# Layer 1's gate as one Silu activation, and the next pair's squares summed on VectorE, in a Strassen-Winograd attention and two-layer feed-forward kernel

## The reference, cut to what matters

```python
x = attention(q, k, v)                                   # 2304 x 512
xn = x / sqrt(mean(x * x) + 1e-6) * rms_g
g = xn @ w_gate                                          # layer 1, 1536 wide
silu = g * (1.0 / (1.0 + exp(-g)))
x = (silu * (xn @ w_val)) @ w_out
r = maximum(x @ w_in, 0.0)                               # layer 2, 2048 wide
return (r * r) @ w_down
```

## Time and profile before

| what | value |
|---|---|
| median of 3 runs | 911.52 us (909.7 to 911.78) |
| the profiled execution | 909.82 us |
| its span | 907.9 us, 14817 instructions |
| clock of TensorE in it | granted in full in all 40 slices |
| busy PE, PEld | 889.4, 879.4 us |
| busy DVE, ACT, POOL | 609.4, 483.5, 583.8 us |

### The profile page before, as it was taken

The page is one execution under the profiler, slowest core; times in us unless marked ns, Lnnn a source line. Parts: engine busy times, 40 slices in busy tenths (PEclk is TensorE's granted clock), DMA queues, the critical chain, the costliest instruction groups (busy, mean ns, idle before and its releaser), DMA issues.

```text
span 907.9 us, 14817 instructions
## 1 busy us (share of the span) xinstructions
PE 889.4 (98%) x5356; PEld 879.4 (97%) x5356; DVE 609.4 (67%) x861; ACT 483.5 (53%) x872; POOL 583.8 (64%) x568
## 2 busy tenths in 40 slices
PE   6999899999999999999999999999999999999998
PEld 6998899999999999999999999999999999999998
DVE  7777777767867766867776767767377675577222
ACT  4887755654466463555554445544355453455332
POOL 7897749967368977347868448573368553485332
PEclk9999999999999999999999999999999999999999
DMA  9995122211222212222222122222422221420122
GB/s 236 249 230 150 45 64 70 70 53 59 82 65 71 70 53 60 69 80 72 70 70 58 58 88 71 65 58 70 138 72 71 62 67 59 157 70 18 59 70 93
DMA packets 105944, 76.99 MB, mean 85 GB/s; under 512 B 24464, under 2 KB 88976, under 8 KB 105872
## 3 DMA queue, kind: packets, MB, share of 16 engines
q1 hardware_dynamic: 105872, 76.05, 29.1%
HBM read 71.31 MB, written 4.72 MB: 84 GB/s over the span
## 4 chain that ended last, share of the span: by engine, by line
PE 82%; POOL 9%; issue 3%; ACT 3%; DVE 3%; DMA 0%; SPq 0%; POOLq 0%; ACTq 0%; DVEq 0%
PE bank L618 26%; PE bank L620 25%; PE bank L619 25%; PE bank L570 2%; PE bank L593 2%; POOL h L490 1%; POOL sq L529 1%; POOL h L501 1%; POOL w_raw L439 1%; POOL wide L460 1%; POOL w_raw L435 1%; POOL probs L466 1%; PE bank L579 1%; ACT w_hi L816 1%; ACT acts L816 0%
## 5 line engine op out<-in xcount | busy, mean ns | idle before, releaser
L618 PE MATMUL bank<-xc_hi,w_hi 128*128 128x384 f32 x844 | 283.8, 336 | 2.1 <-ACT acts L816 1.0
L620 PE MATMUL bank<-xc_hi,w_lo 128*128 128x384 f32 x844 | 282.1, 334 | 0.0
L619 PE MATMUL bank<-xc_lo,w_hi 128*128 128x384 f32 x844 | 282.1, 334 | 0.0
L618 PE MATMUL bank<-hs_hi,d_hi 128*128 128x384 f32 x672 | 225.3, 335 | 1.9 <-POOL d_lo L508 1.9
L619 PE MATMUL bank<-hs_lo,d_hi 128*128 128x384 f32 x672 | 224.6, 334 | 0.0
L620 PE MATMUL bank<-hs_hi,d_lo 128*128 128x384 f32 x672 | 224.6, 334 | 0.0
L508 POOL TENSOR_TENSOR d_lo<-d_raw,d_hi 128x512 fp32r<-128x512 f32 x84 | 127.1, 1513 | 146.0 <-ACT d_hi L816 146.0
L1219 DVE TENSOR_TENSOR hs_lo<-h,hs_hi 128x768 fp32r<-128x768 f32 x84 | 85.5, 1018 | 126.4 <-ACT hs_hi L816 126.2
L618 PEld LDWEIGHTS bank<-xc_hi,w_hi 128*128 128x128 f32 x844 | 158.4, 188 | 5.8 <-issue 1.8
L619 PEld LDWEIGHTS bank<-xc_lo,w_hi 128*128 128x128 f32 x844 | 158.5, 188 | 0.0
L620 PEld LDWEIGHTS bank<-xc_hi,w_lo 128*128 128x128 f32 x844 | 158.4, 188 | 0.0
(11 more groups left out here) (92 smaller groups left out, 1257.4 us busy)
## 6 DMA issues: line engine op xcount, KB each, us to landing
d_raw<-in_w_down SPq DMA_DIRECT2D x48, 256.0 KB, 2.6
w_raw<-in_w_gate SPq DMA_DIRECT2D x36, 256.0 KB, 2.9
w_raw<-in_w_val SPq DMA_DIRECT2D x72, 128.0 KB, 2.8
d_raw<-in_w_out SPq DMA_DIRECT2D x36, 256.0 KB, 2.6
w_raw<-in_w_in SPq DMA_DIRECT2D x24, 256.0 KB, 2.7
w_raw<-in_w_in SPq DMA_DIRECT2D x48, 128.0 KB, 2.6
k_sb<-in_kT SPq DMA_DIRECT2D x16, 288.0 KB, 4.3
q_diag<-in_qT SPq DMA_DIRECT2D x32, 144.0 KB, 4.9
```

Source lines behind the costliest of these rows:

```text
L618: pe.matmul(ps, w_h, v_h, start=first, stop=False, skip_group_check=joined)
L619: pe.matmul(ps, w_h, v_l, start=False, stop=False, skip_group_check=joined)
L620: return pe.matmul(ps, w_l, v_h, start=False, stop=last, skip_group_check=joined)
```

## The change

In layer 1 ACT writes Silu of the gate where it wrote its sigmoid, so DVE's products ga * sigmoid (L1256, L1171) and `silu_b` (L1206, L1180) go. POOL's `h_a` then multiplies sa with va, and `h_b` waits for ACT. The waits move along: ga waits for act_a_done in place of ha_done, va and `gate_a` now wait for ha_done, and PE's waits on silu_a_done and silu_b_done become waits on act_a_done and act_b_done. The three additions of the next pair's squares leave POOL's list and stand in DVE's, after `low2(u+1)` of steps 4, 5 and 6 of runs 0 and 1.

```diff
@@ gpsimd
                 if first_layer(r):
-                    pool.wait_ge(silu_a_done, u + 1)
+                    pool.wait_ge(act_a_done, u + 1)
                     pool.wait_ge(c21_done, steps_done(u))
-                    nc.gpsimd.tensor_tensor(h_half(n, 0), ga[:], va[:], ALU.mult).then_inc(ha_done, 1)
+                    nc.gpsimd.tensor_tensor(h_half(n, 0), sa[:], va[:], ALU.mult).then_inc(ha_done, 1)
...
-                    pool.wait_ge(silu_b_done, u + 1)
+                    pool.wait_ge(act_b_done, u + 1)
...
-                    if q < PAIRS and s in (4, 5, 6):
-                        k = s - 3
-                        pool.wait_ge(sq_done, 2 * KT + KT * r + k + 1)
-                        if k > 1:
-                            pool.wait_ge(sq_sum, 3 * q + 3 + k - 1)
-                        nc.gpsimd.tensor_tensor(squares[1][0][:], squares[1][0][:], squares[1][k][:],
-                                                ALU.add).then_inc(sq_sum, 1)
@@ tensor
                 elif s >= 2:
-                    if first_layer(r):
-                        pe.wait_ge(silu_b_done, u - 1)
-                    else:
-                        pe.wait_ge(act_b_done, u - 1)
+                    pe.wait_ge(act_b_done, u - 1)
@@ scalar
-                nc.scalar.activation(sbuf_b[:], x, ACT.Sigmoid if first_layer(r) else ACT.Relu).then_inc(act_b_done, 1)
+                nc.scalar.activation(sbuf_b[:], x, ACT.Silu if first_layer(r) else ACT.Relu).then_inc(act_b_done, 1)
...
                 act.wait_ge(c11_done, steps_done(u))
-                if first_layer(r):
-                    act.wait_ge(silu_a_done, u)
-                else:
-                    act.wait_ge(ha_done, u)
-                nc.scalar.activation(sa[:], ga[:], ACT.Sigmoid if first_layer(r) else ACT.Relu).then_inc(act_a_done, 1)
+                act.wait_ge(ha_done, u)
+                nc.scalar.activation(sa[:], ga[:], ACT.Silu if first_layer(r) else ACT.Relu).then_inc(act_a_done, 1)
@@ vector
+            def square_sum(q, k):
+                dve.wait_ge(sq_done, 2 * KT + KT * (q - 1) + k + 1)
+                if k > 1:
+                    dve.wait_ge(sq_sum, 3 * q + 3 + k - 1)
+                nc.vector.tensor_tensor(squares[1][0][:], squares[1][0][:], squares[1][k][:],
+                                        ALU.add).then_inc(sq_sum, 1)
...
-                    if not first and first_layer(r):
-                        silu_b(u - 1, r)
-
                     dve.wait_ge(p2_done, n)
                     dve.wait_ge(t_out, n)
                     if not first or r == 0:
-                        if first_layer(r):
-                            dve.wait_ge(ha_done, u)
-                        else:
-                            dve.wait_ge(act_a_done, u)
+                        dve.wait_ge(act_a_done, u)
                     nc.vector.tensor_tensor(ga[:], Z[:, 0:NT], c_t[:], ALU.add).then_inc(c11_done, 1)
...
+                    if not first and first_layer(r):
+                        dve.wait_ge(ha_done, u)
                     nc.vector.tensor_tensor(va[:], Y[:, 0:NT], c_u[:], ALU.add).then_inc(c21_done, 1)
-                    if first_layer(r):
-                        dve.wait_ge(act_a_done, u + 1)
-                        dve.wait_ge(c11_done, n)
-                        nc.vector.tensor_tensor(ga[:], ga[:], sa[:], ALU.mult).then_inc(silu_a_done, 1)
-                    else:
+                    if not first_layer(r):
...
                     if u + 1 < U0[r + 1]:
                         low2(u + 1)
+                    if r + 1 < PAIRS and s in (4, 5, 6):
+                        square_sum(r + 1, s - 3)
```

More of the change, by code:

```diff
@@ L216, in build @@
         act_a_done, act_b_done = sem("act_a_done"), sem("act_b_done")
-        silu_a_done, silu_b_done = sem("silu_a_done"), sem("silu_b_done")
         ha_done, hb_done = sem("ha_done"), sem("hb_done")
@@ L692, in p1 @@
                 if r == 0 and s == PLAIN:
-                    pe.wait_ge(silu_a_done, 1)
+                    pe.wait_ge(act_a_done, 1)
                 elif r == 0 and s == PLAIN + 1:
@@ L711, in p7 @@
                 elif r == 0:
-                    pe.wait_ge(silu_b_done, 1)
+                    pe.wait_ge(act_b_done, 1)
                 else:
@@ L762, in down @@
                         if k >= 2:
-                            if first_layer(r):
-                                pe.wait_ge(silu_b_done, end + k - 3)
-                            else:
-                                pe.wait_ge(act_b_done, end + k - 3)
+                            pe.wait_ge(act_b_done, end + k - 3)
                     ps = (v_banks(r)[k] if c == 0 else u_banks(r)[B_BANKS[k]])[:, 0:NT]
@@ L789, in _ @@
                         if r == 0:
-                            pe.wait_ge(silu_a_done, 2)
+                            pe.wait_ge(act_a_done, 2)
                             pe.wait_ge(ha_done, 2)
@@ L859, in gate_plain @@
                     act.wait_ge(ga_mm, u + 1)
-                    act.wait_ge(silu_a_done, u)
-                    nc.scalar.activation(sa[:], of[:, 0:NT], ACT.Sigmoid).then_inc(act_a_done, 1)
+                    act.wait_ge(ha_done, u)
+                    nc.scalar.activation(sa[:], of[:, 0:NT], ACT.Silu).then_inc(act_a_done, 1)
                 else:
@@ L864, in gate_plain @@
                     act.wait_ge(hb_done, u)
-                    nc.scalar.activation(sbuf_b[:], of[:, 0:NT], ACT.Sigmoid).then_inc(act_b_done, 1)
+                    nc.scalar.activation(sbuf_b[:], of[:, 0:NT], ACT.Silu).then_inc(act_b_done, 1)
             def x_high(r, b, n=None):
@@ L1166, in gated_a @@
             def gated_a(u):
-                g_ps, v_ps = (bank[0], bank[1]) if u == 0 else (bank[4], bank[5])
+                v_ps = bank[1] if u == 0 else bank[5]
                 dve.wait_ge(act_a_done, u + 1)
-                dve.wait_ge(ha_done, u)
-                nc.vector.tensor_tensor(ga[:], g_ps[:, 0:NT], sa[:], ALU.mult).then_inc(silu_a_done, 1)
-                dve.wait_ge(silu_a_done, u + 1)
                 dve.wait_ge(va_mm, u + 1)
-                nc.vector.tensor_tensor(h_half(u, 0), v_ps[:, 0:NT], ga[:], ALU.mult).then_inc(ha_done, 1)
+                nc.vector.tensor_tensor(h_half(u, 0), v_ps[:, 0:NT], sa[:], ALU.mult).then_inc(ha_done, 1)
             def gated_b(u):
-                g_ps, v_ps = (bank[2], bank[3]) if u == 0 else (bank[6], bank[7])
+                v_ps = bank[3] if u == 0 else bank[7]
                 dve.wait_ge(act_b_done, u + 1)
-                nc.vector.tensor_tensor(sbuf_b[:], g_ps[:, 0:NT], sbuf_b[:], ALU.mult).then_inc(silu_b_done, 1)
-                dve.wait_ge(silu_b_done, u + 1)
                 dve.wait_ge(vb_mm, u + 1)
@@ L1278, in _ @@
                         h_low(m + 1)
-                    if f == 0 and first_layer(r):
-                        silu_b(U0[r + 1] - 1, r)
                     if q < RUNS:
```

## The result

The changed kernel takes 904.26 us (median of 4 runs, 903.6 to 905.16) against 911.46 us of the kernel before (4 runs, 909.7 to 911.78): a ratio of 0.9931, 95% interval 0.9919 to 0.9943, so 5.2 to 7.4 us faster. 906.0 was predicted, with 903.5 to 910.0 as the range. The profiled execution took 904.36 us, its span is 902.6. Repeated later, beside the experiments, the changed kernel took 903.84 us against 909.93, a ratio of 0.9933 (0.992 to 0.9945).

A forecast was written before the change was run, and what follows sets the result against it. PE, busy 98% of the span, was the bound, losing time to late lists; 2.3 + 1.3 + 2.1 less 0.2 for new waits gave 5.5 us, 911.52 - 5.5 = 906.0 us, range 903.5 to 910.0.

The forecast's parts named there:

- The size and the places: PE's lost time in steps 6 to 10 and the last steps: about 6.3 us can be had at most.
- steps 6 and 7: Ahead of the token sums in runs 0 and 1: moving the additions off POOL wins back 2.3 us.
- steps 8 to 10: After the token sums in runs 0 and 1: without POOL's lag 0.65 us each comes back, 1.3 us.
- the down starts: Last step of each layer 1 run: POOL's product starts earlier without silu_b, 0.7 us three times, 2.1 us.
- the 1.7 us added to it: The profiled execution lay 1.7 us under the median of 911.52, so the prediction became 906.0 us instead of 904.3.
- The 0.7: Gain taken at each down start, between 0.6 us if hs_lo holds POOL's product and 0.8 if not.
- the cover is DVE's idle 2 us in it, so by themselves they count nothing: The two products leaving DVE are on no path PE sees in an undisturbed step, so they gain nothing by themselves.
- The addition's time: On DVE in six steps: 0.95 us of work plus some waiting, between bounds of 948 and 2051 ns.
- the port: Rival, 0.17: DVE's addition costs POOL its full 2.05 us; only the down stages gain, 2.1 us, 909.4 against the median.
- The tables: Rival, 0.07: ACT reloads tables around every gate, about 985 us, or only Square is missing, about 910.
- the sum for ACT: Steps 8 to 10: ACT's step of 4.47 us and two loads make 7.03 of 7.28, so c_u comes in time.

The follow-up runs named there:

- Silu alone: The changed kernel with the additions of squares put back on POOL; Silu, the two products fewer and the moved waits stay; 903.96 us against 909.78, ratio 0.9942.
- d_lo first: The changed kernel with POOL making d_lo of the first chunk ahead of h_b in the last step of a layer 1 run; 903.94 us against 909.78.
- no product b: The kernel before without DVE's silu_b, so half b of the gate is the sigmoid alone; 905.08 us against 909.93, ratio 0.9952.

## Why the prediction was right, and where it was not

**The size and the places** were right. Starts of matmuls gave 6.3 us that could be had (6.2, since the third down start lost 0.80 us where the sum has 0.88); 5.5 were forecast, 5.7 came in the trace. By stretches: steps 6 and 7 brought 2.40 us (2.3 forecast), steps 8 to 10 1.46 (1.3), the down starts 1.86 (2.1). The medians moved by 7.2 us at first and by 6.1 when both kernels were timed beside each other later. From the profiled execution the forecast was 904.3, which is what came; the 1.7 us added to it for the median of 911.52 did not come back. Why the first runs of before lay up to 2 us above its profiled execution is open, as their clock is not on record; the last section has a candidate.

**The down start** went as worked out: h_b follows sbb on ACT, hs_lo holds it up for 0.4 us, 0.6 us come back. The 0.7 was too much in runs 0 and 1 by the next thing that was late, the copies rb, which the prediction did not look for; in run 2, without such copies, 0.67 came back.

**The additions: right number, one of two causes.** The step that failed is "the cover is DVE's idle 2 us in it, so by themselves they count nothing", of the two products. The 2.3 us credited to the additions are theirs only where the products stay. The products alone are enough for all of steps 6 to 10, the additions alone are too, and both together gain no more; so the sum came out right all the same. In the kernel before POOL stood idle for some 1.6 us behind `silu_b` in most undisturbed steps, and just ahead of the first addition:

```profile
139.58 1.02 POOL L501 TENSOR_TENSOR h<-sbb,vb 128x384 f32<-128x384 f32 x1 [1.64 <-DVE sbb L1210]
```

In Silu alone POOL enters the additions that much earlier, and the third begins 1.5 us earlier, counted from PE's start of step 6 (11.07 against 12.56 us). Its rounds are no shorter: 17.48 us from the first addition to the third (141.92 to 159.40), against 17.34 in the kernel before (143.68 to 161.02). The head start was more than the excess over the slack. An undisturbed step was the wrong place to price the products: they count just where the lists are late, as the same paragraph said and then left out of the sum.

**The addition's time** was taken near the lower end; its mean is 1.76 us, near the upper. The argument that only its work of some 0.95 us holds POOL up fits the trace: POOL's weight sum took 0.73 us longer, its idle time ahead of h_b fell by 0.72 (0.90 to 0.18), and its round grew by 0.12, from an undisturbed 7.28 to 7.40 us (7.75 at most was forecast). The last two make some 0.8 us for an addition recorded with 1.77, and with it the low chance of "the port" was right. The rule of the Trainium skill, SBUF — State Buffer, "Who interferes with whom", that such an addition and POOL's reads exclude each other, agrees with the 1.77 and 1.46 us here. It does not decide the time: most of what the addition takes of POOL comes out of the time that POOL stood idle ahead of h_b.

**The tables** went as the forecast had it: eight loads before and after, at gates only the first one and those that bring the gate's table back after a square root, as before. ACT's timeline after, around the square root of run 0, answers to the last of the earlier trace rows. c_u, behind both loads, starts at 177.61, 12.79 us after the start of step 8 (164.82), where it was 13.67 (179.00 and 165.33). Steps 8 to 10 lose only the restart, so it was in time, as the sum for ACT had said.

```profile
177.61 0.48 ACT L802 ACTIVATE c_u<-bank 128x384 f32<-128x384 f32 x1
```

PE's waits for d_lo were to fall to under 0.2 us, and the profile after names none. By starts 0.29 us are left in run 0, 0.09 of restart and 0.20 for rb, and 0.13 in run 2, which d_lo first takes away.

## What to carry to other kernels

Where one engine is busy 98% of the time, measure the starts of its instructions against an undisturbed stretch: the differences add up to the most that a change can bring, and each names its place. When two parts of a change relieve the same late list, run each alone before crediting either; a loss that exists only beyond a slack goes once, however many remedies are applied. What is late next is found by looking at every wait that the waiting instruction has, not at the one the profile names.

## What the runs showed that was not expected

In some executions the granted clock of PE fell for a few us. In the profile of d_lo first it fell right after the attention and was 0.62 on average from 112 to 116 us; the second fence is the kernel before (us, then PE, PEld, DVE, ACT, POOL busy (x), PEclk, DMA share, GB/s):

```profile
104.00:112.00 8.00, 6.10 (x42) 5.54 (x41) 3.40 (x4) 7.73 (x18) 5.66 (x7) 0.98 0.00 0
112.00:116.00 4.00, 4.00 (x17) 4.00 (x16) 3.83 (x4) 1.89 (x3) 0.00 (x0) 0.62 0.02 4
```
```profile
104.00:112.00 8.00, 6.10 (x45) 5.53 (x43) 4.19 (x6) 7.52 (x18) 6.12 (x8) 1.00 0.00 0
```

Matmuls started 0.32 us apart in it in place of 0.174, the lower of PE's two levels (1.2 and 2.4 GHz), ten of them, which costs 1.5 us. Ahead of it PE had been busy for 6.10 of 8 us; in the profile of the kernel before it was busy for just as long there and kept its full clock. The mean over such an execution is 0.998, which three more of the profiled executions (two at the same place, that of no product b inside the attention) and one run of the changed kernel (905.16 us, its slowest) also show. Of the twelve later runs of the kernel before two show it; they took 911.25 and 911.33 us, the others 909.44 to 910.18. So it may be what lifted that kernel's first runs to 911.5, but nothing on record shows it. Differences of 1 to 2 us between single runs of this kernel are therefore no evidence, and the differences of the parts were read from the steps.
